# Keys stored in tile-aligned ranges, and the two heads' score and value products on halves of TensorE's array

## The reference

```python
block, window = (32, 16)
k_sum = k.reshape(B, H, nb, block, D).max(axis=3)
v_sum = v.reshape(B, H, nb, block, D).mean(axis=3)
scores_l = scale * np.matmul(q, k.transpose(0, 1, 3, 2))
mask_l = np.abs(pos[:, None] - pos[None, :]) < window
scores_s = scale * np.einsum('bhsd,bhnd->bhsn', q, k_sum)
scores_s = scores_s + np.log(block)
scores_l_m = np.where(mask_l, scores_l, -1000000000.0)
scores_all = np.concatenate([scores_l_m, scores_s], axis=-1)
scores_all = scores_all - np.max(scores_all, axis=-1, keepdims=True)
a = np.exp(scores_all)
a = a / (np.sum(a, axis=-1, keepdims=True) + 1e-09)
return np.matmul(a, np.concatenate([v, v_sum], axis=2))
# then: gate = sigmoid(causal 5-tap convolution of x); x = gate * (x @ w_val) @ w_out
# then: u, v = split(relu(x @ w_in)); v = normalised; v = w_spatial @ v + b; out = (u * v) @ w_out2
```

## Time and profile before

| what | us |
|---|---|
| median of 3 runs | 357.35 (356.35 to 358.55) |
| span of the profiled execution | 357.2 |
| PE busy | 320.7 (90%) |
| DVE busy | 233.7 (65%) |
| ACT busy | 150.7 (42%) |
| POOL busy | 136.4 (38%) |
| mean granted TensorE clock | 0.986 of full |

### The profile page before, as it was taken

How to read it: one execution, slowest core, us unless ns; L and a number is a source line. 1 busy time by engine, 2 the same in 40 slices (tenths; PEclk the granted TensorE clock), 3 DMA queues, 4 the chain that set the end, 5 groups by cost and what they waited for, 6 DMA issues and landing times.

```text
span 357.2 us, 5495 instructions
## 1 busy us (share of the span) xinstructions
PE 320.7 (90%) x1876; PEld 292.6 (82%) x1876; DVE 233.7 (65%) x638; ACT 150.7 (42%) x416; POOL 136.4 (38%) x118
## 2 busy tenths in 40 slices
PE   8777967775778899996999999999999999999997
PEld 7666856765668788985799999988889999998886
DVE  6799999999999999979888200028886633331000
ACT  3375656664677676363322322243333211112222
POOL 5219367339434212599205700004444933331000
PEclk9899899999999999999899999999999999999999
DMA  8896774266331221233100000011211000001222
GB/s 180 143 212 146 164 167 108 62 157 143 91 87 50 57 67 59 73 119 89 46 0 1 2 0 2 0 44 46 73 30 31 29 2 0 0 2 59 88 109 98
DMA packets 49721, 25.33 MB, mean 71 GB/s; under 512 B 44170, under 2 KB 44446, under 8 KB 49310
## 3 DMA queue, kind: packets, MB, share of 16 engines
q1 hardware_dynamic: 49694, 24.99, 27.7%
HBM read 21.24 MB, written 3.15 MB: 68 GB/s over the span
## 4 chain that ended last, share of the span: by engine, by line
PE 56%; DVE 23%; issue 10%; POOL 5%; DMA 3%; SPq 1%; ACT 1%; DVEq 0%; POOLq 0%
PE psum L592 52%; DVE probs L858 6%; DVE neg_s L839 6%; DVE gate L901 3%; POOL g_lo L458 2%; DMA v_blk<-in_v_dram 2%; DVE sums_eps L847 2%; POOL win_v_lo L458 2%; DVE k_max L871 1%; DVE recip L852 1%; PE psum L675 1%; DVE k_a L880 1%; POOL win_u_lo L458 1%; PE psum L544 1%; DMA raw<-in_moe_w_in_dram 1%
## 5 line engine op out<-in xcount | busy, mean ns | idle before, releaser
L858 DVE TENSOR_SCALAR probs<-probs,recip 128x184 f32<-128x184 f32 x96 | 60.9, 675 | 1.7
L718 ACT ACTIVATE probs<-neg_s,neg_max 128x184 f32<-128x184 f32 x96 | 42.2, 441 | 44.8 <-DVE neg_max L839 44.5
L458 POOL TENSOR_TENSOR g_lo<-work,g_hi 128x384 fp32r<-128x384 f32 x32 | 36.3, 1147 | 46.8 <-ACT g_hi L819 25.8
L544 PE MATMUL psum<-ident,probs 128*128 128x128 f32 x144 | 25.8, 288 | 22.4 <-DVE probs L858 22.1
L901 DVE SCALAR_TENSOR_TENSOR gate<-xT,conv_c,gate 128x384 f32<-128x384 f32 (+8 forms) x44 | 41.7, 956 | 1.3
L544 PEld LDWEIGHTS psum<-ident,probs 128*128 128x128 f32 x144 | 16.0, 143 | 29.4 <-DVE probs L858 28.7
L458 POOL TENSOR_TENSOR vn_lo<-work,vn_hi 128x512 fp32r<-128x512 f32 x12 | 15.5, 1293 | 57.2 <-DVE vn_hi L1040 57.2
L839 DVE CUSTOM_DVE_ANT_0 neg_s<-psum,mask 128x184 f32<-128x184 f32 x96 | 29.2, 340 | 0.0
L1018 DVE TENSOR_TENSOR wsp_lo<-psum,wsp_hi 128x384 fp32r<-128x384 f32 x12 | 6.6, 548 | 33.6 <-ACT wsp_hi L800 33.6
L458 POOL TENSOR_TENSOR x_lo<-xT,x_hi 128x768 fp32r<-128x768 f32 x8 | 15.0, 1869 | 32.2 <-DVE x_hi L863 32.2
L1050 DVE TENSOR_TENSOR work<-psum,b_row 128x384 f32<-128x384 f32 x16 | 8.9, 558 | 27.8 <-PE psum L592 26.2
(11 more groups left out here) (125 smaller groups left out, 791.3 us busy)
## 6 DMA issues: line engine op xcount, KB each, us to landing
k_nat<-in_k_dram SPq DMA_DIRECT2D x16, 192.0 KB, 3.2
q_nat<-in_q_dram SPq DMA_DIRECT2D x16, 192.0 KB, 3.3
v_blk<-in_v_dram SPq DMA_DIRECT2D x4, 768.0 KB, 7.6
out_dram<-work SPq DMA_DIRECT2D x11, 256.0 KB, 2.0
v_main<-in_v_dram SPq DMA_DIRECT2D x16, 160.0 KB
raw<-in_moe_w_spatial_dram SPq DMA_DIRECT2D x6, 384.0 KB, 3.0
raw<-in_moe_w_out_dram SPq DMA_DIRECT2D x8, 256.0 KB, 2.7
raw<-in_moe_w_in_dram SPq DMA_DIRECT2D x8, 256.0 KB, 2.9
```

The lines of the kernel that those rows point to most:

```text
L458: nc.gpsimd.tensor_tensor(dst_lo, src, dst_hi.bitcast(F32), ALU.subtract).then_inc(lo_sem, 1)
L544: ins = nc.tensor.transpose(bank_t(i)[:, n * P:(n + 1) * P], probs[:, i % 4, c:c + P], ident[:, :])
L718: ins = nc.scalar.activation(probs[:, i % 4, w], neg_s[:, i % 3, w], ACT.Exp, bias=neg_max[:, i % 4, h:h + 1], scale=-1.0, accum_out=sums[ ...
L858: ins = nc.vector.tensor_scalar(a, a, recip[:, i % 4, h:h + 1], None, ALU.mult)
```

## The change

Each key tile gets a range of its own in one buffer, `k_win`, of 240 columns: 16 keys to the left, 16 to the right and 24 maxima for head A, then the 128 main keys, then the same three for head B. Head B's range of 184 columns starts at the first column and head A's ends at the last (`KEYS`), so that both share the main keys and neither needs zeros: each head's score product now reads only its own 64 rows, on one half of the array's rows. ScalarE writes the turned keys straight into the main parts. GpSimd copies the 16-key sides from the neighbouring tiles, with two copies a pair of heads (`k_tails`), and VectorE copies the maxima with one. `own`, `kT`, `k_a` and `k_b` go. The values are loaded as they lie (`v_nat`), and the main value products of the two heads use 64 columns of the array each, and write partitions 0 to 63 and 64 to 127. The rest product uses 112 rows. The scores of the two heads now use three banks in turn, and turned probabilities one.

```diff
-    WIN = P + 2 * WINDOW
-    HEAD = WIN + NB
-    SUM_A, SUM_B, WIN_B, SC = WIN, WIN + NB, WIN + 2 * NB, 2 * HEAD
-
-    MAIN_A, MAIN_B, REST = 0, SC - P, P - WINDOW
-    ROW_TAIL_A, ROW_SUM_A, ROW_SUM_B, ROW_TAIL_B = 16, 48, 72, 96
+    SIDE = 2 * WINDOW + NB
+    HEAD, SC, WIDE = P + SIDE, 2 * (P + SIDE), P + 2 * SIDE
+    MAIN, LEFT, RIGHT, SUMS = SIDE, 0, WINDOW, 2 * WINDOW
+    KEYS = (slice(MAIN, WIDE), slice(0, HEAD))
+    MAIN_A, REST, MAIN_B = 0, P, P + 2 * SIDE
...
-        def bank_s(i):
-            return psum[:, i % 2, :]
-
-        def bank_t(i):
-            return psum[:, 2 + i % 2, :]
+        def bank_s(i, h):
+            return psum[:, (2 * i + h) % 3, 0:HEAD]
+
+        bank_t = psum[:, 3, 0:3 * P]
...
+                for h in range(2):
+                    x = v_h[2 * p + h].rearrange("(t r) d -> r t d", r=P)
+                    d, row = slice(h * D, (h + 1) * D), h * SIDE
+                    sp.dma_start(v_nat[:, s, :, d], x).then_inc(done, 16)
+                    sp.dma_start(v_rest[row + LEFT:row + LEFT + WINDOW, s, 1:T, d],
+                                 x[P - WINDOW:P, 0:T - 1, :]).then_inc(done, 16)
+                    sp.dma_start(v_rest[row + RIGHT:row + RIGHT + WINDOW, s, 0:T - 1, d],
+                                 x[0:WINDOW, 1:T, :]).then_inc(done, 16)
...
-            def k_heads(p):
+            def k_tails(p):
 
                 pool.wait_ge(kT_ready, p + 1)
                 s = p % 2
                 if p >= 2:
                     pool.wait_ge(scores_ready, T * (p - 1))
-                nc.gpsimd.tensor_tensor(k_a[:, s, :, 0:WIN], windows(kT), own[:, 0:1].broadcast_to((P, T, WIN)),
-                                        ALU.mult)
-                nc.gpsimd.tensor_tensor(k_b[:, s, :], kT[:, :], own[:, 1:2].broadcast_to((P, S + 2 * WINDOW)),
-                                        ALU.mult).then_inc(k_heads_ready, 1)
...
+                nc.gpsimd.tensor_copy(sides(p, 1, T - 1, LEFT, WINDOW),
+                                      twice(k_win[:, s, 0:T - 1, MAIN + P - WINDOW:MAIN + P]))
+                nc.gpsimd.tensor_copy(sides(p, 0, T - 1, RIGHT, WINDOW),
+                                      twice(k_win[:, s, 1:T, MAIN:MAIN + WINDOW])).then_inc(k_tails_ready, 1)
...
-                if i >= 2:
-                    pe.wait_ge(masked, i - 1)
-                lhs = qT[:, s, t * P:(t + 1) * P]
-                o = bank_s(i)
-                nc.tensor.matmul(o[:, 0:WIN_B], lhs, k_a[:, s, t, :], start=True, stop=True)
-                nc.tensor.matmul(o[:, WIN_B:SC], lhs, k_b[:, s, t * P:t * P + WIN], start=True,
-                                 stop=True).then_inc(scores_ready, 1)
+                if i >= 1:
+                    pe.wait_ge(masked, 2 * i - 1)
+                for h in range(2):
+                    d = slice(h * D, (h + 1) * D)
+                    ins = nc.tensor.matmul(bank_s(i, h), qT[d, s, t * P:(t + 1) * P], k_win[d, s, t, KEYS[h]],
+                                           start=True, stop=True)
+                ins.then_inc(scores_ready, 1)
...
-                nc.tensor.matmul(o, v_main[:, s, t, 0:P], pT[:, 0:P], start=True, stop=False)
-                nc.tensor.matmul(o, v_main[:, s, t, D:D + P], pT[:, P:2 * P], start=False, stop=False)
-                nc.tensor.matmul(o, v_rest[:, s, t, :], pT[:, 2 * P:3 * P], start=False,
-                                 stop=True).then_inc(x_summed, 1)
+                nc.tensor.matmul(o[0:D], v_nat[:, s, t, 0:D], pT[:, 0:P], start=True, stop=False,
+                                 skip_group_check=True)
+                nc.tensor.matmul(o[D:P], v_nat[:, s, t, D:P], pT[:, P:2 * P], start=True, stop=False,
+                                 skip_group_check=True)
+                nc.tensor.matmul(o, v_rest[0:2 * SIDE, s, t, :], pT[0:2 * SIDE, 2 * P:3 * P], start=False, stop=True,
+                                 skip_group_check=True).then_inc(x_summed, 1)
...
-                for h, n in enumerate((SUM_A, SUM_B)):
-                    ins = nc.vector.tensor_scalar(k_a[:, p % 2, :, n:n + NB],
-                                                  k_max[:, :].rearrange("p (a n) -> p a n", a=1).broadcast_to(
-                                                      (P, T, NB)), own[:, h:h + 1], None, ALU.mult)
+                sums_of = k_max[:, :].rearrange("p (a n) -> p a n", a=1)
+                ins = nc.vector.tensor_copy(sides(p, 0, T, SUMS, NB), twice(sums_of.broadcast_to((P, T, NB))))
...
-            nc.vector.memset(v_main[:, :, :, :], 0.0).then_inc(v_zeros, 1)
...
-            nc.vector.tensor_scalar(k_a[:, 0, :, 0:WIN], windows(kT), own[:, 0:1], None,
-                                    ALU.mult).then_inc(k_heads_ready, 1)
```

More of the change, by code:

```diff
@@ L100, in attention_gated_mlp @@
             qT = sb("qT", [P, 2, S], F32, att)
-            v_main = sb("v_main", [P, 2, T, 3 * D], F32, att)
+            v_nat = sb("v_nat", [P, 2, T, P], F32, att)
         wu_hi = sb("wu_hi", [P, C, DM], F32R)
@@ L108, in attention_gated_mlp @@
             with ExitStack() as att:
-                kT = sb("kT", [P, S + 2 * WINDOW], F32, att)
-                k_a = sb("k_a", [P, 2, T, WIN_B], F32, att)
-                k_b = sb("k_b", [P, 2, S + 2 * WINDOW], F32, att)
-                own = sb("own", [P, 2], F32, att)
+                k_win = sb("k_win", [P, 2, T, WIDE], F32, att)
                 k_max = sb("k_max", [P, NB], F32, att)
@@ L117, in attention_gated_mlp @@
                 v_mean = sb("v_mean", [4 * NB, 2, D], F32, att)
-                mask = sb("mask", [P, 3, SC], F32, att)
+                mask = sb("mask", [P, 3, WIDE], F32, att)
                 neg_s = sb("neg_s", [P, 3, SC], F32, att)
@@ L203, in attention_gated_mlp, with sides, twice @@
         stored = [sem(f"stored{i}") for i in range(3)]
-        def windows(x):
-            w = x[:, 0:WIN]
-            return bass.AP(w.tensor, w.offset, [list(w.ap[0]), [P, T], [1, WIN]])
+        def sides(p, first, tiles, n, count):
+            w = k_win[:, p % 2, first, n:n + count]
+            return bass.AP(w.tensor, w.offset, [list(w.ap[0]), [WIDE, tiles], [HEAD, 2], [1, count]])
+        def twice(x):
+            return bass.AP(x.tensor, x.offset, [list(x.ap[0]), list(x.ap[1]), [0, 2], list(x.ap[2])])
         def k_step(p):
             return 1 if p == 0 else 0
-        def bank_s(i):
-            return psum[:, i % 2, :]
-        def bank_t(i):
-            return psum[:, 2 + i % 2, :]
+        def bank_s(i, h):
+            return psum[:, (2 * i + h) % 3, 0:HEAD]
+        bank_t = psum[:, 3, 0:3 * P]
         bank_qk = psum[:, 4:6, :].rearrange("p a n -> p (a n)")
@@ L276, in wait_bank @@
                 nc.tensor.wait_ge(taken, m + 1)
-            elif g < 2:
-                nc.tensor.wait_ge(masked, STEPS - 1 + g)
+            elif g < 3:
+                nc.tensor.wait_ge(masked, 2 * STEPS - 2 + g)
             elif g in (4, 5):
@@ L575, in keep_warm @@
                 for _ in range(n):
-                    nc.tensor.transpose(psum[:, 7, 0:P], ident[:, :], ident[:, :])
+                    nc.tensor.transpose(psum[:, 3, 2 * P:3 * P], ident[:, :], ident[:, :])
             pe.wait_ge(ident_ready, 1)
@@ L752, in _ @@
             turned_k(0)
-            turned(0, qT[:, 0, :], q_turned, qT_ready)
+            turned_q(0)
             act.wait_ge(conv_turned, 1)
@@ L768, in _ @@
                 if t == 3 and p + 1 < PAIRS:
-                    turned(p + 1, qT[:, (p + 1) % 2, :], q_turned, qT_ready)
+                    turned_q(p + 1)
                 if t == 3 and 1 <= p <= W_OUT:
@@ L838, in mask_scores @@
                 w = slice(h * HEAD, (h + 1) * HEAD)
-                ins = nc.vector.tensor_tensor_reduce(
-                    out=neg_s[:, i % 3, w], in0=bank_s(i)[:, w], in1=mask[:, e, w], scale=-(float(D) ** -0.5),
-                    scalar=BIG, op0=ALU.add, op1=ALU.min, accum_out=neg_max[:, i % 4, h:h + 1])
-                if h == 1:
-                    ins.then_inc(masked, 1)
+                nc.vector.tensor_tensor_reduce(
+                    out=neg_s[:, i % 3, w], in0=bank_s(i, h), in1=mask[:, e, KEYS[h]], scale=-(float(D) ** -0.5),
+                    scalar=BIG, op0=ALU.add, op1=ALU.min, accum_out=neg_max[:, i % 4, h:h + 1]).then_inc(masked, 1)
             def add_eps(i):
```

111 lines of the change are left out of this document (46 added, 65 removed).

## The result

| kernel | median us | runs | ratio to the kernel before, 95% interval |
|---|---|---|---|
| before | 357.4 (356.35 to 358.55) | 4 | |
| changed | 343.35 (340.56 to 344.29) | 4 | 0.9586 (0.9545 to 0.9626) |

The changed kernel is 14.0 us faster.

A forecast was written before the change was run, and what follows sets the result against it. VectorE, held by GpSimd's products, was taken to bound attention; 357.2 - 18.4 + 2.8 + 1.5 - 1.4 + 2.0 - 0.3 = 343.4, so the forecast was 343.5 us, range 334 to 354.

The forecast's parts named there:

- The bound and the removed term: In attention VectorE sets the pace; removing GpSimd's two products for seven pairs of heads gives -18.4 us.
- The copies: GpSimd's two copies per pair of heads delay VectorE 0.4 us, seven times: +2.8 us, bounds 0 and +4.9.
- The block sums: GpSimd's block sums of v start some 3 us earlier and can hold the normalising: +1.5 us, bounds -1 and +3.
- VectorE's own instructions: One copy of the block maxima per pair replaces two on VectorE: -1.4 us, bounds -1.6 and 0.
- TensorE: Attention steps with array halves and switches take about 1.95 us on TensorE: +2.0 us, bounds 0 and +6.
- One bank less ahead: Scores wait for the first head's mask one step back, with one bank for turned probabilities: costs nothing by itself.
- The tail: At the end of attention, where TensorE bounds three value groups: -0.3 us, up to 0.7 us won.
- The signs: Attention 12 to 17 us shorter, start unchanged, two normalisings below 1 us more than 0.54, TensorE's transposes still waiting for probabilities.
- The stall: Copies and earlier block sums hold VectorE as long as the products in half the pairs: about 350 us, chance 0.10.
- DMA: DMA becomes the bound in the first half, giving back up to 5 us: 348.5 us, chance 0.07.
- The third rival: TensorE becomes the bound through switches without overlap: 358.6 or 380 us; chance 0.09 for over 1% slower, 0.09 within 1%.
- The fourth, the clock: In attention TensorE idles more and runs at 1.2 GHz, 2.60 us a step: no gain, 357 us, chance 0.03.

The follow-up runs named there:

- Experiment 1: Kernel before, with GpSimd making only the first 160 columns of k_a and k_b from the second pair of heads: 339.4 us, ratio 0.9516.
- Experiment 2: Changed kernel with GpSimd multiplications of 960 and 800 columns on an unused tile put back for each pair but the first: 361.5 us, ratio 1.0117.
- Experiment 4: Changed kernel without GpSimd's two side-key copies from the second pair on, one small memset in their place: 341.5 us, ratio 0.9580.
- experiment 5: Changed kernel with fewer switches: main values on all columns 341.0 us, rest product first 340.2, no halves 339.0; changed kernel as it is beside them 343.5.
- Experiment 3: Kernel before, with scores waiting for the mask, and turned probabilities for the copy, of step i-1 instead of i-2: 359.9 us, ratio 1.0076.

## Why the prediction was right, point by point

**The bound and the removed term.** VectorE set the pace and was held by GpSimd's products at seven places: -18.4. Experiment 1 shows 17.7 of it with TensorE's work untouched. Experiment 2 takes 18.2 the other way, with 13.1 us more of holds and 6.4 more of waits for scores, so it does not confirm the whole term.

**The copies.** +2.8 was taken between 0 and 4.9. GpSimd's copies take 0.31 to 0.53 us each, about what the product's rate suggested, but at the seven places two normalisings take 0.68, 0.66, 0.65, 0.54, 0.66, 0.60 and 0.66 us, so the term is 0.7. Experiment 4 finds no clear difference. At 43.17 us, for example, two normalisings start inside two copies that run from 43.10 to 43.71, and take 0.65 us, only 0.11 more than undisturbed. The Trainium skill (SBUF — State Buffer, § Who interferes with whom) says the pair is locked for the whole of an instruction, and that who issues first gets it. The rows agree that a copy costs VectorE something, 0 to 0.14 us a place, but they do not show a hold for a copy's whole length, nor the 0.7 a place behind the 4.9.

**The block sums** were put at +1.5. Two of the three cases hold VectorE about as long as before. In the third the normalisings take 2.63 us and `sums_eps` 0.80, where the earlier trace rows had 1.79 with 1.08 for the normalisings behind it: 2.09 + 0.64 against 1.63 + 0.54, so +0.6. The DMA of the block now decides in all three cases when they start (before, in the first two): GpSimd waits 19.8 us for it in three waits, at no cost to VectorE.

**VectorE's own instructions.** The one copy of the maxima takes 0.31 us instead of 0.50 for two; the -1.4 was right. The start did not move: the first mask is at 12.87 us, and was at 12.85. The load that it waits for did not land sooner.

**TensorE.** Here the steps were least secure. The prediction had 1.30 a step if the halves overlap, and it did not know the switch; it chose 0.1 us a switch and an overlap in part, 1.95 together with the turns. The trace shows a full overlap and 0.17 to 0.21 a switch: 1.78 + 0.22 = 2.00. Two errors cancelled. The charge of +2.0 is what VectorE's wait for scores was in the profiled execution (2.1 us), but by experiment 5 the halves cost 4.5 us in all, within the bounds of 0 and +6 and above the value taken. The working given for the upper bound does not make 6: 0.24 on half of 48 steps is 5.8, and the same again would be 11.5. The Trainium skill (TensorEngine Tiling (Array Packing), § Key Properties) states that tiles execute in parallel and that a change of the tiling mode drains TensorE. The trace agrees with the first by the starts 0.01 us apart, and its pauses of 0.17 to 0.21 us at the changes fit the second.

**One bank less ahead** was said to cost nothing by itself. That step failed. Experiment 3 measures 2.9 us on the kernel before. The reasoning compared an undisturbed step of VectorE with the length of the scores. What counts, by the waits there, is what is queued behind the scores: after a held normalising TensorE starts later and the transposes come later still. Without the long holds the price is smaller. The kernel without halves also has one bank less ahead and is as fast as experiment 1, which has both banks (339.0 and 339.4 us), with 1.4 us less work on the maxima; by these medians about 1 us is left for the bank, an estimate within the spread.

**The tail.** -0.3 was taken for the last value products. From the last normalising to the end it is 215.2 us in both, so nothing was won. That the switches took it is likely, since TensorE is the bound there, but no run shows it.

**The sum** by the rows of the changed kernel is -18.4 + 0.7 + 0.6 - 1.4 + 2.1 = -16.4, against -15.5 between the two spans; 0.9 us is not accounted for. That 343.5 met 343.35 so closely is luck in part. The copies and block sums were put 3.0 us too high, and what the halves and the lost bank cost was put too low. And the sum mixes two measures. It starts from a span, 357.2, and reads it as the median of the times, 357.35. In every execution with both on record the time is 1.7 to 1.9 us above the span (343.46 and 341.7 for the changed kernel's profile). By this the profile of before belongs to an execution of about 359.0 us, 1.6 above the median, which accounts for the spans differing by 15.5 and the medians by 14.0. As a span, the predicted 343.4 was 1.7 above the measured 341.7.

**The signs.** Attention is 15.5 us shorter, the start stays, two normalisings at the seven places take at most 0.14 more than 0.54, and the pauses without a semaphore are there. One sign of being right failed: TensorE's transposes no longer wait for the probabilities; the wait has moved to the scores, for the mask.

**The rivals.** The stall did not move, and DMA did not bind VectorE. The third rival, TensorE as the bound, did not decide. Its price of a switch was near, 0.22 against the measured 0.17 to 0.21; its condition, no overlap, did not hold. The fourth, the clock, was given 0.03 with the argument that the idle stretches go. Its outcome, no gain at all, did not come. But the argument was incomplete: the two profiles of the changed kernel at 0.94 and 0.93 have 14 and 16 us of attention at 1.2 GHz, against 7 to 8 before, and experiment 2 has 44. A stall that stays came ahead of such a stretch. In the changed kernel the block sums hold a pair of normalisings at 74.61 for 2.63 us, TensorE is busy 0.19 and 0.44 of the microseconds from 76 and from 77, and from 79 to 85 the clock is at 0.50:

```profile
76.00:77.00 1.00, 0.19 (x2) 0.00 (x0) 1.00 (x1) 0.00 (x0) 1.00 (x1) 1.00 0.79 186
77.00:78.00 1.00, 0.44 (x4) 0.30 (x4) 1.00 (x6) 0.19 (x1) 0.92 (x2) 1.00 0.83 188
78.00:79.00 1.00, 1.00 (x10) 0.58 (x8) 0.97 (x3) 1.00 (x5) 0.92 (x2) 0.98 1.12 248
79.00:80.00 1.00, 0.70 (x2) 0.41 (x2) 0.96 (x4) 1.00 (x3) 0.84 (x3) 0.50 0.97 210
```

## What to carry to other kernels

Read the duration of the same instruction across the trace, not the busy share. An engine at 98% can be standing in a quarter of it, and the release may be work moved off another engine, not a faster matmul. When two edits come in one change, undo each alone: here the halves of the array cost 2 to 4.5 us, and the new layout of the keys (no zeros to write) gave nearly 18. With four switches for eight products a step, the halves lose more in the pauses than they gain by working at the same time. That they would pay where many products in the same mode follow each other is what these prices suggest; no run here tried it.

## What the runs showed of the hardware that I had not expected

- Going between the whole array and halves of its rows or columns costs 0.17 to 0.21 us at 2.4 GHz and 0.33 to 0.41 us at 1.2 GHz, in the profiles of the changed kernel, seen as a pause without a semaphore ahead of the next weight load.
- Two float32 products on the two column halves, issued one behind the other, start 0.01 us apart and take 0.20 us together where they took 0.45, and two score products of 184 columns on the row halves take 0.30 us together, as long as one on the whole array.
- Kernels with halves mostly run more of attention at the lower clock: their mean there is 0.83 to 0.97 in seven profiles. Without halves it is 0.97 before, 0.99 and 1.00 in three others, but 0.92 in experiment 3. TensorE's busy time does not explain it: 98 of 114 us with the rest product first at a clock of 0.90, 104 in the changed kernel at 0.93, 99 without halves at 1.00. Filling TensorE's time with transposes went with a rise from 0.94 to 0.97. Whether it is the smaller amount of work in the array or the pauses that lets the clock fall wasn't tried.
